# A two-expert-stage kernel on one core: the first stage's down product in seven products instead of eight

## What is computed

```python
# 1: decayed linear attention
state = gamma * state + k_t (outer) v_t;   y_t = scale * q_t @ state
# 2: gated feed-forward, d_ff = 1536
xn = x / rms(x) * rms_g
x = (silu(xn @ w_gate) * (xn @ w_val)) @ w_out
# 3: four experts, d_ff = 1024 each, weighted by p = domain_probs / sum
out = sum over e of p[:, e] * (relu(x @ w1[e]) @ w2[e])
```

## Time and profile before

| | |
|---|---|
| median of 3 runs | 844.16 us (844.03 to 844.45) |
| profiled execution, own time | 844.63 us |
| its span | 842.8 us |
| granted TensorE clock | full in all 40 slices |
| attention and start | to about 83 us |
| step 2 | about 83 to 350 us |
| step 3 | the rest |

### The profile page before, as it was taken

How to read it: one execution, slowest core, us unless ns; L and a number is a source line. 1 busy time by engine, 2 the same in 40 slices (tenths; PEclk the granted TensorE clock), 3 DMA queues, 4 the chain that set the end, 5 groups by cost and what they waited for, 6 DMA issues and landing times.

```text
span 842.8 us, 12814 instructions
## 1 busy us (share of the span) xinstructions
PE 832.8 (99%) x4846; PEld 772.2 (92%) x4846; DVE 470.0 (56%) x776; ACT 242.3 (29%) x483; POOL 408.1 (48%) x460
## 2 busy tenths in 40 slices
PE   8999999999999999999999999999999999999998
PEld 8888999999999998889999989889899898898997
DVE  4598555545455548774554555545545545545545
ACT  3676222222322325422222222222212212222221
POOL 3998835446372639832736336326326325425100
PEclk9999999999999999999999999999999999999999
DMA  9801010100110010101101100100110110110003
GB/s 348 324 24 51 26 51 26 51 26 26 45 32 26 26 51 26 51 1 51 51 9 42 51 18 34 51 32 19 51 45 5 51 51 2 51 51 1 25 14 137
DMA packets 12875, 43.15 MB, mean 51 GB/s; under 512 B 1424, under 2 KB 1808, under 8 KB 12816
## 3 DMA queue, kind: packets, MB, share of 16 engines
q1 hardware_dynamic: 12528, 41.69, 14.1%
q10 hardware_dynamic: 288, 0.65, 0.2%
HBM read 39.19 MB, written 3.15 MB: 50 GB/s over the span
## 4 chain that ended last, share of the span: by engine, by line
PE 91%; DVE 2%; POOL 2%; DMA 2%; ACT 1%; issue 1%; SPq 1%; DVEq 0%
PE bank L525 29%; PE bank L524 29%; PE bank L526 29%; DMA ring<-qkv 2%; PE bank L473 1%; PE bank L466 1%; POOL w_lo L346 1%; PE bank L453 1%; POOL x_lo L241 0%; DVE x_all L941 0%; DVE x_lo L241 0%; ACT x_hi L713 0%; DVE x_sum L237 0%; PE bank L503 0%; POOL wd_lo L365 0%
## 5 line engine op out<-in xcount | busy, mean ns | idle before, releaser
L524 PE MATMUL bank<-x_hi,w_hi 128*128 128x384 f32 x784 | 264.4, 337 | 2.7 <-ACT u L718 1.1
L526 PE MATMUL bank<-x_lo,w_hi 128*128 128x384 f32 x784 | 263.2, 336 | 0.0
L525 PE MATMUL bank<-x_hi,w_lo 128*128 128x384 f32 x784 | 263.2, 336 | 0.0
L1048 DVE SCALAR_TENSOR_TENSOR out_acc<-bank,p_norm,out_acc 128x512 f32<-128x512 f32 (+1 forms) x181 | 135.0, 746 | 127.5 <-PE bank L526 127.1
L524 PEld LDWEIGHTS bank<-x_hi,w_hi 128*128 128x128 f32 x784 | 147.4, 188 | 10.6 <-issue 5.1
L525 PEld LDWEIGHTS bank<-x_hi,w_lo 128*128 128x128 f32 x784 | 147.3, 188 | 5.5
L526 PE MATMUL bank<-wd_lo,h_hi 128*128 128x512 f32 (+1 forms) x386 | 152.1, 394 | 0.0
L525 PE MATMUL bank<-wd_hi,h_lo 128*128 128x512 f32 (+1 forms) x386 | 151.7, 393 | 0.0
L524 PE MATMUL bank<-wd_hi,h_hi 128*128 128x512 f32 (+1 forms) x386 | 150.0, 389 | 0.5 <-DVE out_acc L1044 0.3
L526 PEld LDWEIGHTS bank<-x_lo,w_hi 128*128 128x128 f32 x784 | 147.2, 188 | 0.0
L346 POOL TENSOR_TENSOR w_lo<-w_raw,w_hi 128x256 fp32r<-128x256 f32 x196 | 142.7, 765 | 3.0 <-ACT w_hi L685 0.8
(11 more groups left out here) (71 smaller groups left out, 877.1 us busy)
## 6 DMA issues: line engine op xcount, KB each, us to landing
w_raw<-wu SPq DMA_DIRECT2D x28, 512.0 KB, 4.4
ring<-qkv SPq DMA_DIRECT2D x23, 512.0 KB, 9.0
wd_raw<-wd SPq DMA_DIRECT2D x22, 512.0 KB, 3.6
...
```

The costliest lines, as they stand in the source:

```text
L524: pe.matmul(dst, s_hi, m_hi, start=first, stop=False, skip_group_check=True)
L525: pe.matmul(dst, s_lo, m_hi, start=False, stop=False, skip_group_check=True)
L526: return pe.matmul(dst, s_hi, m_lo, start=False, stop=last, skip_group_check=True)
L1048: nc.vector.scalar_tensor_tensor(out=to, in0=new, scalar=p, in1=to, op0=ALU.mult, op1=ALU.add).then_inc(posted, 1)
```

## The change

The down product of step 2 is done in seven products as well, for the first ten of its twelve pairs `r` (`RP` = 10). The 2 x 2 blocks are the two hidden blocks by two token halves (A) and the two halves of each weight row block (B); a product now is two **parts** (`down1`) of 3 matmuls, one for each 128 output columns, in banks 6 and 7. M1, M6, M7, M4 and then M5, M3 build on the same bank, so each part is posted (14 per pair) before the next product goes on in it. The hidden blocks go into SBUF (`h1_raw`, `h1_a21`), four sums are made of them on VectorE (`hidden_sum`), and seven blocks are split in four groups (`hidden_hi(r, g)` on ScalarE, `hidden_lo(r, g)` on VectorE, for the first pair in part on GpSimd). The down weights get four sums and seven splits on GpSimd (`split_wd`; for block 0 in part on VectorE and ScalarE, and its low parts after the parts of x). The tuples of counts now have a place after each product: the parts of a pair stand after M7, M4 and M3 of the next unit and after M5, M6, M2 and M7 of the one behind it. The last two pairs keep the tiles of 6 matmuls (`tile1`, `hidden_hi3`, `hidden_lo3`, `post3`). In units 1 to 3, M1 is done during the unit before. The arena of SBUF is larger, for which the scratch of the DMAs is made smaller. In the lists around the start and the end of step 2 a few operations change places, one part of x (S3 of half 2) moves to GpSimd.

```diff
+DOWNS = (("M1", "A11", "B11", True, (0, 0)), ("M6", "S2", "T2", False, (1, 0)), ("M7", "S3", "T3", False, (1, 1)),
+         ("M4", "A22", "T4", False, (0, 1)), ("M2", "A12", "B21", True, (0, 0)), ("M5", "S1", "T1", True, (1, 1)),
+         ("M3", "S4", "B22", False, (1, 0)))
+HS = {"A11": 0, "S2": 1, "S3": 2, "A22": 3, "A12": 4, "S1": 5, "S4": 6}
+GROUPS = (slice(0, 1), slice(1, 3), slice(3, 5), slice(5, 7))
+GROUP_OF = {"A11": 0, "S2": 1, "S3": 1, "A22": 2, "A12": 2, "S1": 3, "S4": 3}
...
+FIRST, SECOND = (0, 0, 0, 0, 2, 2, 2), (0, 2, 2, 2, 2, 0, 0)
+EARLY, LATE = (0, 0, 0, 0, 0, 0, 0), (2, 2, 2, 2, 2, 2, 2)
 TILES1 = [(0, 0), (1, 0), (0, 1), (1, 1), (2, 1), (3, 1), (2, 0), (3, 0)]
-FIRST, SECOND = (0, 1, 2), (2, 1, 2)
-EARLY, LATE = (0, 0, 2), (2, 2, 2)
-END0, END1 = (0, 2, 2), (2, 1, 1)
-NEXT0, NEXT1 = (0, 1, 2, 2), (3, 0, 0, 0)
+END0, END1 = (0, 0, 0, 2, 2, 0, 0), (0, 2, 0, 1, 1, 0, 0)
+NEXT0, NEXT1 = (0, 0, 0, 1, 2, 0, 2), (0, 3, 0, 0, 0, 0, 0)
+TILES, TILES_NEXT = (0, 1, 0, 1, 2, 0, 2), (0, 0, 0, 2, 2, 0, 2)
...
+    return PARTS * min(r, RP) + T1N * max(0, r - RP)
...
+            def split_wd(d):
+                i = d % 2
+                sum_wd_13(d)
+                sum_wd_24(d)
+                pool.wait_ge(wd_sums, 4 * d + 4)
+                nc.gpsimd.tensor_scalar(wd_hi[i][:, :, :], wd_raw[i][:, 0:7, :], 1.0, 1.0,
+                                        ALU.mult, ALU.mult).then_inc(wd_hi_ready, 1)
+                split_wd_lo(d, 0)
+            def split_wd_lo(d, first):
+                i = d % 2
+                pool.wait_ge(wd_hi_ready, d + 1)
+                if first:
+                    pool.wait_ge(wd_ready, NP * d + first)
+                for _, _, ws, _, _ in DOWNS[first:]:
+                    nc.gpsimd.tensor_tensor(wd_lo[i][:, WS[ws], :], wd_raw[i][:, WS[ws], :],
+                                            wd_hi[i][:, WS[ws], :].bitcast(F32), ALU.subtract).then_inc(wd_ready, 1)
...
+            split_wd_lo(0, 1)
+            hidden_lo(0, 2)
+            hidden_lo(0, 3)
...
+            def down1(r, i):
+                n, p, s = first_part(r) + i, r // J, i % 2
+                _, xs, ws, first, _ = DOWNS[i // 2]
+                pe.wait_ge(wd_ready, wd_count(p, i // 2))
+                pe.wait_ge(hid_split[GROUP_OF[xs]], r + 1)
                 if n == 0:
                     pe.wait_ge(x_normal, 16)
                 elif n >= 2:
                     pe.wait_ge(posted, n - 1)
+                c = slice(P * s, P * s + P)
+                mm = three(bank[6 + s][:, 0:TB], wd_hi[p % 2][:, WS[ws], c], wd_lo[p % 2][:, WS[ws], c],
+                           h1_hi[:, HS[xs], :], h1_lo[:, HS[xs], :], first, True)
+                mm.then_inc(down_done, 1)
...
+            def unit(q, k=None, r=None, first=0, downs=(0,) * NP, tiles=(0,) * NP):
+                c, j = UNITS1[q] if q < Q1 else (F1 + UNITS2[q - Q1][0], UNITS2[q - Q1][1])
+                for place in range(NP):
+                    if not (place == 0 and q in (1, 2, 3)):
+                        product(q, c, j, k, PRODUCTS[place][0])
+                    if place == 4 and q in (0, 1, 2):
+                        product(q + 1, UNITS1[q + 1][0], UNITS1[q + 1][1], (None, 1, None)[q], "M1")
+                    if q == 0 and place == 0:
+                        sum_squares(2)
+                    elif q == 0 and place == 2:
+                        sum_squares(3)
+                    for i in range(sum(downs[:place]), sum(downs[:place + 1])):
+                        if r < RP:
+                            down1(r, first + i)
+                        else:
+                            tile1(r, first + i)
...
+            unit(3, None, 0, sum(EARLY), LATE)
+            for r in range(1, RP):
+                unit(2 * r + 2, None, r, 0, FIRST)
+                unit(2 * r + 3, None, r, sum(FIRST), SECOND)
...
+            def hidden_hi(r, g):
+                if g == 2:
+                    act.wait_ge(hid_ready, 4 * r + 4)
+                else:
+                    act.wait_ge(hid_sums, 4 * r + (1, 2, None, 4)[g])
+                nc.scalar.activation(h1_hi[:, GROUPS[g], :], h1_raw[:, GROUPS[g], :], ACT.Copy).then_inc(hid_hi_ready[g], 1)
...
+                r = q // 2 - 1
+                if q % 2 == 0:
+                    hidden_hi(r, 1)
                 copy_up(q, "M6", u2)
+                if q % 2 == 0:
+                    hidden_hi(r, 2)
+                else:
+                    hidden_hi(r + 1, 0)
                 silu(q, 0)
                 copy_up(q, "M7", u3)
+                if q % 2 == 0:
+                    hidden_hi(r, 3)
                 silu(q, 1)
-                hidden_hi(q, 1)
-                if q + 1 < Q1:
-                    copy_up(q + 1, "M1", m1)
-                hidden_hi(q, 0)
+                copy_up(q + 1, "M1", m1)
...
+                    to = y if q >= QP else h1_raw[:, HS["A22"], :] if v else h1_a21[:, :]
...
+            def hidden_sum(r, to):
+                a21, a11, a12, a22 = (h1_a21[:, :] if n == "A21" else h1_raw[:, HS[n], :] for n in ("A21", "A11", "A12", "A22"))
+                s2, s3 = h1_raw[:, HS["S2"], :], h1_raw[:, HS["S3"], :]
+                x, y, op, blocks, sums = {"S3": (a11, a21, ALU.subtract, 2, 0), "S2": (a22, s3, ALU.subtract, 3, 1),
+                                          "S4": (a12, s2, ALU.subtract, 4, 2), "S1": (a21, a22, ALU.add, 3, 0)}[to]
+                dve.wait_ge(hid_ready, 4 * r + blocks)
+                if sums:
+                    dve.wait_ge(hid_sums, 4 * r + sums)
+                nc.vector.tensor_tensor(h1_raw[:, HS[to], :], x, y, op).then_inc(hid_sums, 1)
+            def hidden_lo(r, g):
+                dve.wait_ge(hid_hi_ready[g], r + 1)
+                dve.wait_ge(hid_sums, 4 * r + (1, 3, 4, 4)[g])
+                nc.vector.tensor_tensor(h1_lo[:, GROUPS[g], :], h1_raw[:, GROUPS[g], :],
+                                        h1_hi[:, GROUPS[g], :].bitcast(F32), ALU.subtract).then_inc(hid_split[g], 1)
...
+            def post1(r, first, last):
+                j = r % J
+                for i in range(first, last):
+                    n, s = first_part(r) + i, i % 2
+                    name, _, _, _, (half, a) = DOWNS[i // 2]
+                    d = 2 * half + s
+                    dve.wait_ge(down_done, n + 1)
+                    to, new = x_all[j][:, d, a, :], bank[6 + s][:, 0:TB]
+                    if r < J and name not in ("M2", "M5", "M3"):
+                        nc.vector.tensor_copy(to, new).then_inc(posted, 1)
+                    else:
+                        dve.wait_ge(posted, n - 1)
+                        nc.vector.tensor_tensor(to, new, to, ALU.add).then_inc(posted, 1)
...
+            def first1(q):
+                r = q // 2 - 1
+                hidden_lo(r, 1)
+                hidden_sum(r, "S1")
+                c11(q)
+                hidden_lo(r, 2)
+                post1(r, 0, 2)
+                c22_sum(q)
+                post1(r, 2, 4)
                 hidden(q, 1)
                 c12(q)
                 hidden(q, 0)
-                hidden_lo(q, 1)
-                hidden_lo(q, 0)
-            def unit1(q, tiles=None, counts=(0, 0, 0)):
-                def some(place):
-                    for i in range(sum(counts[:place]), sum(counts[:place + 1])):
-                        post1(tiles[0], tiles[1], tiles[2] + i)
-                some(0)
+                post1(r, 4, 6)
+                hidden_sum(r + 1, "S3")
+            def second1(q):
+                r = q // 2 - 1
+                post1(r, 6, 8)
+                hidden_lo(r, 3)
+                post1(r, 8, 10)
                 c11(q)
-                some(1)
+                hidden_lo(r + 1, 0)
+                post1(r, 10, 12)
                 c22_sum(q)
-                some(2)
-                hidden_all(q)
+                post1(r, 12, 14)
+                hidden(q, 1)
+                hidden_sum(r + 1, "S2")
+                c12(q)
+                hidden(q, 0)
+                hidden_sum(r + 1, "S4")
...
+    nc = bacc.Bacc("TRN2", target_bir_lowering=False, num_devices=1, dynamic_dma_scratch_size=2048)
```

More of the change, by code:

```diff
@@ L278, in _ @@
                     load_wd(0)
-            for p in range(1, F1 // 2):
+            for p in range(1, D1):
                 load_w(2 * p)
@@ L633, in _ @@
-            unit1(4 * end + 2, None, (end, 0, 0), END0)
-            unit1(4 * end + 3, None, (end, 0, sum(END0)), END1)
-            def unit2(q, k=None, first=0, counts=(0, 0, 0, 0), tiles=(1, 1, 2, 2)):
-                f, j = UNITS2[q - Q1]
-                c = F1 + f
-                def some(place):
-                    for i in range(sum(counts[:place]), sum(counts[:place + 1])):
-                        tile1(end, 1, first + i)
+            def unit(q, k=None, r=None, first=0, downs=(0,) * NP, tiles=(0,) * NP):
[14 more added lines that the diff above has]
+                            tile1(r, first + i)
@@ L661, in _ @@
+            unit(Q1, 2, F1 - 1, 0, NEXT0)
```

(75 more changed lines are left out.)

408 lines of the change are left out of this document (215 added, 193 removed).

## The result

The changed kernel takes 847.44 us (847.23 to 848.11, 6 runs), the kernel before in the same job 844.45 us (844.03 to 844.78, 6 runs): ratio 1.0037, 95% interval 1.0026 to 1.0047, slower by 3.0 us. The changed kernel's profiled execution took 848.11 us, span 846.3, against 844.63 and 842.8 before.

The account below looks back on a forecast made before the run. TensorE's matmul count times 0.1733 us was taken as the bound in the first expert's loop. Against 844.63 us: -10.4 + 9.2 + 1.5 + 3.5 + 0.5 = +4.3, so 848.9, brought to the median 848.5 us; range 836 to 855.

Parts of the forecast that it names:

- The gain: Down products of step 2, ten pairs: 60 matmuls less at 0.1733 us each, 10.4 us saved, all on the path.
- First units: First unit of a pair: VectorE, disturbed by GpSimd, brings `c11` late; M4 stalls 1.15 us, 9.2 us in all (0 to 15).
- eight such units: Loop, r = 1 to 8: the first unit of every pair was to lose the 1.15 us stall before M4.
- The full lock: First units: a wait behind GpSimd's split can reach 1.7 us; five units lose another 0.8, some 4 us more.
- Second units: Second unit of a pair: 0.35 us to spare before the part due at 8.32; 1.5 us over nine units (0 to 5).
- The start: Units 2 to 4: GpSimd late with weight block 3, 3.5 us of TensorE waiting, plus 0.5 us in unit 2.
- the single wait of 2 to 5 us: Sign for the start: TensorE waits once for `w_lo` near 108 us.
- my undisturbed 109.7: Start: time in us at which block 3 is usable if nothing disturbs GpSimd; TensorE asks for it at 108.0.
- Attention: Attention stage: costed at nothing; VectorE's four `wd` sums take 2.2 us at most.
- Rival 3: Loop: VectorE becomes the bound, 23.7 us per pair, total 854.4 us; chance 0.14, with the full-lock variant.

Follow-up runs that it names:

- run 12: Run 10 with ScalarE splitting `w_hi` of weight blocks 5, 7 and 9, and GpSimd splitting B11 and T1 of block 3 earlier: 838.87 us, ratio 0.994.
- run 1: The changed kernel with ScalarE's copy of M7 put ahead of silu: 843.80 us, ratio 0.9995 to the kernel before.
- run 4: The changed kernel with GpSimd's 1792-column split of every weight block cut into seven of 256: 856.03 us, ratio 1.014.
- run 3: The changed kernel with the x sum S4 of the second token half moved from GpSimd to VectorE: 845.29 us, ratio 1.0013.
- run 10: Run 7 with, at the start, S4 and a hidden split moved from GpSimd to VectorE and posts put earlier: 843.29 us, ratio 0.9989, in two groups.
- runs 6: Run 1 plus, on VectorE in first units, `c11` ahead of S1 and two posts ahead of the split of A22 and A12: 846.22 us, ratio 1.0028.
- 7: Run 6 with `c22_sum` also ahead of the split of A22 and A12: 846.98 us, ratio 1.0028.
- run 11: Run 10 with the split of A22 and A12 behind the third and fourth post: 844.09 us, ratio 0.9988.

## Why the prediction was right, and where it was not

The forecast, 848.5 us and slower, came true at 847.44. The mechanism, VectorE held by GpSimd ahead of `c11` and GpSimd late at the start, is there; that the number is so near is luck, as the sum below shows. Its terms against what was measured:

- **The gain, -10.4**: right. 60 matmuls fewer, and undisturbed (run 12) two pairs take 43.68 us instead of 45.76, 12 x 0.1733 less.
- **First units, +9.2**: mechanism right, size 5.8. The chain `c11`, silu, copy of M7, M4 is shown by run 1. The waits on that copy are 0.47, 0.57, 1.35, 1.44, 1.55 and 0.41 us (r = 1, 2, 3, 5, 7 and 9). The step that failed is "eight such units": GpSimd does not disturb each pair, it holds VectorE in every second one and is idle in the other. Within one hit unit (r = 3, 5, 7) the sizes were off too: S2 and S4 waited 0.05 to 0.24 us where I took 0.3 each, S1 0.54 (0.6 taken), and the split 1.32 where I took 0.4 and had bounded any one wait by 0.82. So there were three waits of about 1.4 us and three small ones, where I had eight of 1.15.
- **The full lock**: the Trainium skill (SBUF — State Buffer, "SBUF: two separate sides") says that whichever starts first, a VectorE instruction with two SBUF inputs or a GpSimd instruction, has the shared ports for its whole length. The traces agree: 2.27 us beside 1.89 us of GpSimd, 1.31 when that is cut in pieces (run 4), 0.96 when it is gone (run 12). I had weighed the rule and gone by the nearest row, a wait of 0.4 us; that row showed the end of a hold, not a price of one. The starts and ends of the same rows could have told me: that split ended 0.81 us after GpSimd's instruction (338.75 against 337.94), exactly as the one of 2.27 us did (152.64 against 151.83). It was short because it had begun 1.16 us into GpSimd's 1.69, not 0.43 into 1.89.
- **Second units, +1.5**: what is left of the 6.8 us without the five larger waits is 1.5 us, but only some 0.95 of it lies where I had it, before the part that is due 8.3 us into the unit, and in four units only (167.9, 213.3, 258.8 and 299.2 us). Another 0.4 is the matmul behind each of the five waits, 0.08 us late. Right in place, a little too large.
- **The start, +4.0** (3.5 for block 3, 0.5 for unit 2): 5.9 us, that is 2.1 and 4.3 less the 0.5 of `c11` above. Block 3 cost 1.1, not 3.5 (the single wait of 2 to 5 us that was to show this term did not come), though it was usable at 113.6, 3.9 us later than my undisturbed 109.7 and about at the upper end that I had given: TensorE asked later, having lost 1.9 us before M4 of unit 2 and 2.2 on low parts and posts. I had walked GpSimd's list and not ScalarE's, where a copy stands behind an operation that waits for GpSimd (run 3).
- **Attention, 0**: the four `wd` sums took 4.10 us, not at most 2.2, again beside GpSimd; the first product of step 2 began at 53.53 instead of 53.36 us. The zero was nearly right, the bound for VectorE was not.
- **Rival 3, VectorE the bound**: it isn't by its total. It is busy 156 of 188 us in the loop, and in run 12, with the list of run 10, TensorE never waits from 130 to 318 us. But in runs 6, 7, 10 and 11 waits stayed: none of the orders tried had room for both holds. One alone may fit: in run 11 only 0.2 us of waits follow the first hold (193.94 us, a split of 2.27) and 0.8 the second (205.44, 2.26), and in run 12 one split of 2.27 us is left, at 278.8 us (r = 9, where the list is another), for which TensorE does not wait at all.

So the sum, +4.3 against a measured +3.5 (-10.4 + 5.8 + 1.5 + 5.9, and 0.7 elsewhere), came out near because a term too large (9.2 for 5.8) and one too small (4.0 for 5.9) went against each other. That is luck.
